# Attention in block turns: two tiles normalised by ScalarE, and the second pair's q and k loaded in four parts

## The chip, the cores and the metric

One core of one Trainium2 chip runs the whole program. The metric is the device time of one execution in microseconds. The kernel before took 1048.01 us in the median of three runs (1047.76 to 1048.04).

## The reference, cut to what matters

Attention with a position bias is followed by two mixture stages. The change lies in the attention alone.

```
scores = q @ k.T / sqrt(64)                       # 4 batches, 8 heads, 576 x 576
x      = log1p(|i-j|) / log1p(max(i,1))           # the bias stage:
bias   = relu(x * w1 + b1) @ w2                   # one 576 x 576 plane for each head
attn   = exp(scores + bias - max);  attn /= sum(attn)
out    = attn @ v                                 # then router, experts, gated FFN
```

## The kernel before, in words

**Bias stage** (`bias_stage`, up to about 65 us). Its 36 steps make 16 query rows each, for all 8 heads. In a step VectorE writes three hidden blocks (line 140) and ScalarE a fourth (line 234), TensorE multiplies them with w2 (line 267), ScalarE copies the product from PSUM into `b_res` (line 244), and SyncE (SP) stores these 288 KB to DRAM (line 151). `b_res` has four buffers: ScalarE's copy of step s waits until the store of step s-4 has landed (`s_st[u]`). On the same SP queue, `loads` issues other transfers at given steps, behind the store of the step: four tiny ones at steps 2, 4, 6 and 8; q and k of the second pair of heads, 576 KB each, both at step 22 (`load_qk(e, 1, 1)`); and two small ones at steps 28 and 30. At steps 10, 18, 26 and 34 SP loads a finished 576 KB tile of the bias back from DRAM (`load_bias`, line 331), after waiting for the stores that wrote it (line 155).

**Attention** (about 64 to 312 us). It runs over 16 pairs of heads. A pair has five slots: slots 0 to 3 hold 128 query rows of either head (h = 0, 1), slot 4 (`MIX`) the last 64 rows of both. For each unit TensorE makes the scores (line 437), VectorE adds the bias and takes the maximum (`add_bias`, line 597), ScalarE takes the exponential with its row sums (line 663), VectorE transposes it in blocks of 32 (`turn`, line 609). One slot later TensorE multiplies with v in four visits (`values`, line 552). ScalarE copies the finished output of a pair out of PSUM (`keep_out`, lines 671 and 677); TensorE turns it back into rows (`turn_back`, line 566), two pairs late, into the PSUM banks of the h = 1 scores; VectorE multiplies it by the reciprocals of the sums (`normal`, line 628), in two halves: tiles 0 and 1 (128x288), then tiles 2 to 4 (128x432). GpSimd adds up the router's part of that (line 508), SP stores the rest.

The order on each engine is written out by hand. In slot 3 of pair p VectorE does: `add_bias` of slot 4, both halves of `normal(p - 2)`, the turns of h = 0 and h = 1; in slot 4: `add_bias` of the next pair's slot 0 for h = 0 and h = 1, the turn of slot 4. TensorE does in slot 3: scores of slot 4, `turn_back(p - 2)`, the last visit of `values(p - 1)`; in slot 4: scores of the next pair's slot 0, h = 0 and h = 1. The scores of h = 1 wait for `s_x`, the semaphore that both halves of `normal` raise, because `turn_back` had used their banks. The pairs 2 to 13 run in a loop of six rounds with two pairs each, the others are written out; in the loop, waits for values that depend on the round need register instructions, and `sem.apart` puts an increment of a spare semaphore (line 87) between such waits.

Of the kernel before, what the change touches and what calls it, by code (L numbers as in the profile page):

```python
# [33 lines left out]
class Sems:  # L34
# [3 lines left out]
    LOOPS = """b_mm b_ev b_st0 b_st1 b_st2 b_st3 a_st00 a_st01 a_st10 a_st11 a_s a_b a_e a_t a_o a_oe a_bk a_r a_x a_pa  # L38
# [237 lines left out]
def front_stages(sem, arena, psum, qt, kt, vt, ww, wg, biasd, xd, ident, rt, small):  # L276
# [35 lines left out]
    s_s, s_b, s_e, s_t, s_o, s_oe, s_bk, s_r, s_x = (  # L312
        sem.loop("a_" + n) for n in ("s", "b", "e", "t", "o", "oe", "bk", "r", "x"))
# [40 lines left out]
    def split_k(e, it, u):  # L354

        pair = it * 2 + u
        e.wait_ge(s_k[u], sem.at(s_k[u], it * 16 + 16))
# [67 lines left out]
    def scores(e, p, u, uses, s, h):  # L425
# [4 lines left out]
        if s == 0 and h == 1 and from_pair(p, 3):  # L430
            e.wait_ge(s_x, sem.at(s_x, p * 2 - 4))
# [13 lines left out]
    def sync(e):  # L445

        def store_first(p, u):
            e.wait_ge(s_x, sem.at(s_x, p * 2 + 1))
# [5 lines left out]
        def store_second(p, u):  # L454
            e.wait_ge(s_x, sem.at(s_x, p * 2 + 2))
# [78 lines left out]
    def tensor(e):  # L534
# [54 lines left out]
    def vector(e):  # L589
# [11 lines left out]
        def turn(p, u, s):  # L601

            unit, n, w = p * TPP + 2 * s, p * SLOTS + s, (u + s) % 2
            if s == 0:
                e.wait_ge(s_o, sem.at(s_o, p - 1))
            for h in range(1 if s == MIX else 2):
                at = P if s == MIX else (P + Q) * h + Q * s
                e.wait_ge(s_e, sem.at(s_e, unit + h + 1))
                t = e.transpose(pt[:, u, :, at:at + Q], pr[:, w, S * h:S * h + S].rearrange("p (k q) -> p k q", q=Q))  # L609
            t.then_inc(s_t, 1)  # L610
# [7 lines left out]
        def normal(p, u, uses, half):  # L618

            n = 2 + half  # L620
            at = (slice(None), u, slice(2 * half, 2 * half + n), slice(None))
            if half == 0:
                e.wait_ge(s_r, sem.at(s_r, p * 2 + 2))
            st = (s_st0, s_st1)[half][u]
            e.wait_ge(s_bk, sem.at(s_bk, p * 2 + half + 1))
            e.wait_ge(st, sem.at(st, uses * (32, 64)[half]))
# [22 lines left out]
        for half in range(2):  # L649
            normal(NPAIR - 2, 0, NPAIR // 2 - 1, half)  # L650
        inverse(NPAIR - 1, 1)
        for half in range(2):
            normal(NPAIR - 1, 1, NPAIR // 2 - 1, half)

    def scalar(e):

        def exps(p, u, uses, s, h):
# [7 lines left out]
            mm.then_inc(s_e, 1)  # L665

# [1165 lines left out]
```

## Time and profile before

| | us |
|---|---|
| median of three runs | 1048.01 |
| the profiled execution | 1048.78 |
| its span, first to last instruction | 1046.9 |
| TensorE busy | 993.2 (95%) |
| VectorE busy | 791.9 (76%) |
| ScalarE busy | 410.0 (39%) |
| GpSimd busy | 203.8 (19%) |

Busy is the time in which an engine executes; the rest of the span it waits. The profiled execution is 0.77 us above the median of the runs, and its span 1.88 us shorter than its own time. Most of the time lies behind the attention, in stages that the change does not touch.

### The profile page before, as it was taken

What the parts mean: (1) busy time and instruction counts of PE and PEld (TensorE: products, weight loads), DVE (VectorE), ACT (ScalarE), POOL (GpSimd) and SP (SyncE); (2) the same over time, 40 slices, a digit from 0 to 9 for tenths busy, and PEclk for the clock granted to TensorE, in tenths of its full rate; (3) what the DMA queues carried; (4) which work ended last, traced back from release to release, by engine and by line L of the source; (5) the groups of instructions that cost most, each with busy time, mean ns of one, the idle gap of its engine ahead of it and who ended that gap; (6) DMA issues with size and microseconds to landing.
All of it is one profiled execution on the core that took longest, in us unless ns stands there. A gap on an engine that the chain in (4) does not pass through costs nothing.

```text
span 1046.9 us, 28553 instructions
## 1 busy us (share of the span) xinstructions
PE 993.2 (95%) x10409; PEld 901.3 (86%) x10410; DVE 791.9 (76%) x1268; ACT 410.0 (39%) x783; POOL 203.8 (19%) x195
## 2 busy tenths in 40 slices
PE   5868899999988999999999999999999999999997
PEld 2347788777877999999999999999999999999996
DVE  8978899999958457757474699787777767777675
ACT  6865555555534346444352352222111121211111
POOL 2035545655502212212120000000100100100101
PEclk9978999999999999999999999999999999999999
DMA  3874757758426816515122620020100100000000
GB/s 136 274 268 196 243 176 245 252 169 284 132 65 203 300 44 213 213 53 212 37 81 69 221 73 1 1 58 26 60 0 13 47 0 30 30 0 0 31 1 31
DMA packets 66797, 117.42 MB, mean 112 GB/s; under 512 B 27104, under 2 KB 38416, under 8 KB 64704
## 3 DMA queue, kind: packets, MB, share of 16 engines
q1 hardware_dynamic: 62720, 103.45, 29.3%
q0 software_dynamic: 4032, 13.37, 3.7%
q8 instruction: 28, 0.46, 0.2%
q14 instruction: 17, 0.14, 0.0%
HBM read 91.41 MB, written 25.40 MB: 112 GB/s over the span
## 4 chain that ended last, share of the span: by engine, by line
PE 68%; DVE 2%; issue 1%; POOL 1%; ACT 1%; DMA 0%; POOLq 0%; DVEq 0%
PE psum L1704 28%; PE psum L1712 14%; PE psum L1217 11%; PE psum L1226 11%; PE psum L1203 1%; PE psum L552 1%; PE psum L437 1%; DVE f_eg L1659 0%; PE psum L1265 0%; PE psum L566 0%; DMA e_xin<-x_tokens,e_col 0%; PE psum L847 0%; DVE r_inq L962 0%; POOL e_xin L1169 0%; POOL e_col L1165 0%
## 5 line engine op out<-in xcount | busy, mean ns | idle before, releaser
L1659 DVE RECIPROCAL f_eg<-f_eg 128x384 f32<-128x384 f32 x72 | 183.4, 2547 | 0.0
L1627 ACT ACTIVATE f_eg<-psum 128x384 f32<-128x384 f32 x72 | 35.5, 492 | 311.9 <-PE psum L1704 311.9
L663 ACT ACTIVATE a_pr<-a_sc,a_nmax 128x576 f32<-128x576 f32 x144 | 110.8, 770 | 96.3 <-DVE a_nmax L597 96.2
L1704 PE MATMUL psum<-f_x,f_ghi 128*128 (+1 forms) x576 | 147.6, 337 | 0.4 <-DVE f_x L1520 0.4
L1704 PE MATMUL psum<-f_x,f_vhi 128*128 (+1 forms) x576 | 146.1, 334 | 0.0
L597 DVE CUSTOM_DVE_ANT_0 a_sc<-psum,a_bias 128x576 f32<-128x576 f32 x144 | 104.3, 752 | 22.7 <-PE psum L437 20.2
L437 PE MATMUL psum<-a_khi,a_qs 128*128 128x288 f32 x320 | 101.1, 336 | 13.8 <-DVE a_nmax L597 13.8
L1704 PEld LDWEIGHTS psum<-f_x,f_ghi 128*128 128x128 f32 x576 | 105.8, 188 | 6.6 <-DVE f_x L1520 0.6
L1596 POOL DMA_INDIRECT out<-f_ob,f_cols x18 | 18.2, 1009 | 464.9 <-ACT f_ob L1613 316.9
L552 PE MATMUL psum<-a_pt,a_v 32*64 32x128 f32 (+1 forms) x4608 | 98.9, 294 | 8.3 <-issue 8.3
L1704 PEld LDWEIGHTS psum<-f_x,f_vhi 128*128 128x128 f32 x576 | 104.0, 188 | 0.0
L609 DVE STREAM_TRANSPOSE a_pt<-a_pr 128x576 f32<-128x576 f32 x144 | 103.9, 756 | 0.0
L1704 PE MATMUL psum<-f_x,f_glo 128*128 (+1 forms) x288 | 97.1, 337 | 0.0
L552 PEld LDWEIGHTS psum<-a_pt,a_v 32*64 32x64 f32 x4608 | 79.6, 131 | 20.1 <-issue 17.9
L1704 PE MATMUL psum<-f_x,f_vlo 128*128 (+1 forms) x288 | 96.2, 334 | 0.0
L1655 DVE TENSOR_SCALAR f_eg<-f_eg 128x384 f32<-128x384 f32 x72 | 26.5, 368 | 88.5 <-ACT f_eg L1627 88.5
L437 PEld LDWEIGHTS psum<-a_khi,a_qs 128*128 128x128 f32 x320 | 62.4, 195 | 34.6 <-DVE a_nmax L597 17.9
L437 PE MATMUL psum<-a_klo,a_qs 128*128 128x288 f32 x320 | 90.9, 304 | 0.0
L1226 PE MATMUL psum<-e_hhi,e_w2hi 128*128 128x288 f32 x288 | 87.4, 303 | 0.0
L1217 PE MATMUL psum<-e_xhi,e_w1hi 128*128 128x288 f32 x288 | 87.1, 303 | 0.0
L1712 PE MATMUL psum<-f_ohi,f_alo 128*128 128x512 f32 x216 | 85.4, 396 | 0.0
L1712 PE MATMUL psum<-f_olo,f_ahi 128*128 128x512 f32 x216 | 85.3, 395 | 0.0
(235 smaller groups left out, 2150.0 us busy)
## 6 DMA issues: line engine op xcount, KB each, us to landing
a_v<-v SPq DMA_DIRECT2D x16, 1152.0 KB, 5.6
e_raw<-ew SPq DMA_DIRECT2D x16, 1024.0 KB, 5.7
bias_ihj<-b_res SPq DMA_DIRECT2D x36, 288.0 KB, 2.6
a_qraw<-q SPq DMA_DIRECT2D x16, 576.0 KB, 4.4
a_kraw<-k SPq DMA_DIRECT2D x16, 576.0 KB, 5.4
a_bias<-bias_ihj SPq DMA_DIRECT2D x16, 576.0 KB, 6.5
xn_t<-e_yn SPq DMA_DIRECT2D x8, 576.0 KB, 3.1
x_tokens<-a_xp SPq DMA_DIRECT2D x64, 64.0 KB, 3.8
```

What stands on the lines that cost most here:

```text
L437: mm = e.matmul(s_ps[:, h, half, 0:HALF], qs[:, u, c:c + P], k[:, u, a * S + half * HALF:a * S + (half + 1) * HALF], start=(i == 0), stop= ...
L552: mm = e.matmul(o_ps[64 * h:64 * h + 64, g, to:to + n], vv[rows, u, k, 64 * h:64 * h + 64], pt[rows, u, k, first:first + n], start=(k == 0 ...
L597: e.tensor_tensor_reduce(sc[:, h, :].rearrange("p (a s) -> p a s", a=2), s_ps[:, h, :, 0:HALF], bias[:, 2 * s + h, :].rearrange("p (c s) - ...
L609: t = e.transpose(pt[:, u, :, at:at + Q], pr[:, w, S * h:S * h + S].rearrange("p (k q) -> p k q", q=Q))
L663: mm = e.activation(pr[:, w, S * h:S * h + S], sc[:, h, :], ACT.Exp, bias=nmax[:, h:h + 1], scale=-1.0, accum_out=sums[:, u, 2 * s + h:2 * ...
L1217: mm = e.matmul(bank[:, 0:BT], w[:, k, :], x[:, u, k, :], start=(k == 0 and n == 0), stop=(k == KD - 1 and n == 2))
L1226: mm = e.matmul(banks.y[:, k, 0:BT], w[:, k * P:(k + 1) * P], h[:, f % 3, :], start=(f == 0 and n == 0), stop=(f == KF - 1 and n == 2))
L1627: e.activation(self.eg[:, k % 2, :], self.g_ps[k % 2][:, 0:CHUNK], ACT.Exp, scale=-1.0).then_inc(self.s_e, 1)
L1655: e.tensor_scalar(x, x, 1.0, None, ALU.add).then_inc(self.s_c, 1)
L1659: e.reciprocal(x, x).then_inc(self.s_c, 1)
L1704: mm = e.matmul(acc[:, 0:CHUNK], a, b, start=(q == 0 and i == 0), stop=(q == KD - 1 and i == 2))
L1712: mm = e.matmul(self.o_ps[t], x, y, start=(f == 0 and i == 0), stop=(f == KFF - 1 and i == 2))
```

## The change

1. `normal` is split between two engines. ScalarE does tiles 0 and 1 as four copies with a scale, one for each tile and head (128x72 each), in slot 3 ahead of the exponential of slot 4. VectorE does tiles 2 to 4 as before, but between the turn of h = 0 and the turn of h = 1 of slot 3; `turn` takes the head as an argument for this. Both reciprocals of `inverse` are kept.
2. `s_x` becomes two semaphores, `s_xf` (ScalarE's part) and `s_xs` (VectorE's). Whoever waited for `s_x` now waits for one or for both: the scores of h = 1 of slot 0 on TensorE, with two more `sem.apart`; `turn_back`; the stores on SP; `add_logits` on GpSimd.
3. In the bias stage q and k of the second pair are loaded in four parts of 288 KB: the halves of k at steps 12 and 14, the halves of q at steps 16 and 20. The waits for them count 32 instead of 16 in the first round.

```diff
-        if step == 22:
-            load_qk(e, 1, 1)
+        if step in (12, 14, 16, 20):
+            i = (12, 14, 16, 20).index(step)
+            part = slice(S * (i % 2), S * (i % 2) + S)
+            if i < 2:
+                e.dma_start(kraw[:, 1, part], kt[1, :, part]).then_inc(s_k[1], 16)
+            else:
+                e.dma_start(qraw[:, 1, i % 2, :], qt[1, :, part]).then_inc(s_q[1], 16)
...
         if s == 0 and h == 1 and from_pair(p, 3):            # TensorE, scores
-            e.wait_ge(s_x, sem.at(s_x, p * 2 - 4))
+            e.wait_ge(s_xf, sem.at(s_xf, p - 2))
+            sem.apart(e, p)
+            e.wait_ge(s_xs, sem.at(s_xs, p - 2))
+            sem.apart(e, p)
...
                 if exists(np_) and ns != MIX:                # VectorE, pair
                     add_bias(np_, nu, nuses, ns, 1)
+                turn(p, u, s, 0)
                 if s == MIX - 1 and from_pair(p, 2):
-                    for half in range(2):
-                        normal(p - 2, u, uses - 1, half)
-                turn(p, u, s)
+                    normal(p - 2, u, uses - 1)
+                if s != MIX:
+                    turn(p, u, s, 1)
...
+        def normal(p, u, uses):                              # ScalarE
+
+            e.wait_ge(s_r, sem.at(s_r, p * 2 + 2))
+            e.wait_ge(s_bk, sem.at(s_bk, p * 2 + 1))
+            e.wait_ge(s_st0[u], sem.at(s_st0[u], uses * 32))
+            e.wait_ge(s_pa, sem.at(s_pa, p - 1))
+            for t in range(2):
+                for h in range(2):
+                    n = 2 * t + h
+                    x = e.activation(xp[:, u, t, h, :], back_ps[0][:, XW * n:XW * n + XW], ACT.Copy, scale=rinv[:, u, n:n + 1])
+            x.then_inc(s_xf, 1)
...
                 np_, nu, nuses, ns = next_of(p, u, uses, s)  # ScalarE, pair
+                if s == MIX - 1 and from_pair(p, 2):
+                    normal(p - 2, u, uses - 1)
                 if s == MIX and from_pair(p, 1):
                     keep_out(p - 1)
```

## Rows read from the trace of the kernel before

**Rows 1.** Page, parts 1 and 4: busy time, and the chain that ended last.

```profile
PE 993.2 (95%) x10409; PEld 901.3 (86%) x10410; DVE 791.9 (76%) x1268; ACT 410.0 (39%) x783; POOL 203.8 (19%) x195
...
PE 68%; DVE 2%; issue 1%; POOL 1%; ACT 1%; DMA 0%; POOLq 0%; DVEq 0%
```

**Rows 2.** Timeline of VectorE in two pairs: start us, us, instruction [idle before].

```profile
183.91 0.74 DVE L609 STREAM_TRANSPOSE a_pt<-a_pr 128x576 f32<-128x576 f32 x1
184.77 0.76 DVE L597 CUSTOM_DVE_ANT_0 a_sc<-psum,a_bias 128x576 f32<-128x576 f32 x1
...
196.25 0.76 DVE L597 CUSTOM_DVE_ANT_0 a_sc<-psum,a_bias 128x576 f32<-128x576 f32 x1 [0.63 <-PE psum L437]
...
197.92 1.43 DVE L609 STREAM_TRANSPOSE a_pt<-a_pr 128x576 f32<-128x576 f32 x2
199.37 0.76 DVE L597 CUSTOM_DVE_ANT_0 a_sc<-psum,a_bias 128x576 f32<-128x576 f32 x1
...
200.73 0.77 DVE L609 STREAM_TRANSPOSE a_pt<-a_pr 128x576 f32<-128x576 f32 x1
```

**Rows 3.** Timeline of TensorE in the same two pairs.

```profile
184.04 0.30 PE L437 MATMUL psum<-a_klo,a_qs 128*128 128x288 f32 x1
...
195.80 1.39 PE L566 MATMUL psum<-a_xw,a_ot 128*128 x10
...
198.63 0.30 PE L437 MATMUL psum<-a_klo,a_qs 128*128 128x288 f32 x1
...
199.16 0.29 PE L437 MATMUL psum<-a_klo,a_qs 128*128 128x288 f32 x1
...
201.89 0.40 PE L552 MATMUL psum<-a_pt,a_v 32*64 32x160 f32 x8 [0.23 <-issue]
```

**Rows 4.** Groups by line and shape, 110 to 300 us: busy, mean ns | idle.

```profile
L628 DVE TENSOR_TENSOR a_xp<-psum,a_rinv 128x432 f32<-128x432 f32 x13 | 7.8, 603 | 0.2
...
L677 ACT ACTIVATE a_ot<-psum 64x64 f32<-64x64 f32 x26 | 5.5, 212 | 0.2
```

**Rows 5.** Timeline of ScalarE in the second of the two pairs.

```profile
197.12 0.78 ACT L663 ACTIVATE a_pr<-a_sc,a_nmax 128x576 f32<-128x576 f32 x1 [1.79 <-DVE a_nmax L597]
...
198.39 0.60 ACT L671 ACTIVATE a_ot<-psum 128x512 f32<-128x512 f32 x1 [0.39 <-PE psum L552]
```

**Rows 6.** ScalarE in the bias stage: waits (total, times, longest), then its timeline.

```profile
ACT b_res L244 <- DMA bias_ihj<-b_res: 5.4, 3, 4.5
...
34.49 0.74 ACT L244 ACTIVATE b_res<-psum,b_invp 128x576 f32<-128x576 f32 x1 [0.53 <-DMA bias_ihj<-b_res]
...
55.12 0.74 ACT L244 ACTIVATE b_res<-psum,b_invp 128x576 f32<-128x576 f32 x1 [4.55 <-DMA bias_ihj<-b_res]
```

**Rows 7.** Line 151, stores issued 14 to 28, at 29.4, 46 to 50.5 us.

```profile
DMA to landing us min/median/max: 2.1/2.1/2.2
...
DMA to landing us min/median/max: 4.9/4.9/4.9
...
DMA to landing us min/median/max: 7.2/8.0/8.9
```

**Rows 8.** Windows: length, busy us of each engine, PEclk, DMA share, GB/s.

```profile
29.00:36.00 7.00, 6.45 (x92) 2.44 (x90) 7.00 (x18) 6.47 (x11) 0.00 (x0) 1.00 0.87 292
36.00:40.00 4.00, 3.67 (x56) 1.30 (x48) 4.00 (x11) 4.00 (x7) 0.00 (x0) 1.00 0.59 226
40.00:56.00 16.00, 10.94 (x152) 3.89 (x144) 15.77 (x37) 11.13 (x18) 0.00 (x0) 1.00 0.86 273
...
71.00:73.00 2.00, 1.39 (x7) 1.04 (x5) 2.00 (x5) 0.94 (x4) 0.62 (x4) 0.50 0.45 114
```

**Rows 9.** Timeline of VectorE in the bias stage.

```profile
12.76 43.01 DVE L140 TENSOR_SCALAR b_hid<-b_table,b_shift 128x576 f32<-128x576 f32 x100
59.21 1.38 DVE L140 TENSOR_SCALAR b_hid<-b_table,b_shift 128x576 f32 x3 [3.44 <-PE psum L267]
```

**Rows 10.** Timeline of VectorE at the end of the attention.

```profile
312.18 0.61 DVE L628 TENSOR_TENSOR a_xp<-psum,a_rinv 128x432 f32<-128x432 f32 x1 [0.22 <-PE psum L566]
```

More of the change, by code:

```diff
@@ L37 @@
     START = 128
-    LOOPS = """b_mm b_ev b_st0 b_st1 b_st2 b_st3 a_st00 a_st01 a_st10 a_st11 a_s a_b a_e a_t a_o a_oe a_bk a_r a_x a_pa
+    LOOPS = """b_mm b_ev b_st0 b_st1 b_st2 b_st3 a_st00 a_st01 a_st10 a_st11 a_s a_b a_e a_t a_o a_oe a_bk a_r a_xf a_xs a_pa
                e_xs e_xt e_xh e_xl e_h e_hh e_hl e_o e_sq e_yc e_pre e_ss e_rt e_inv e_ys e_st e_fold
@@ L311, in front_stages @@
     s_sp, s_kk, s_qh, s_ql, s_low = sem("a_sp"), sem("a_kk"), sem("a_qh"), sem("a_ql"), sem("a_low")
-    s_s, s_b, s_e, s_t, s_o, s_oe, s_bk, s_r, s_x = (
-        sem.loop("a_" + n) for n in ("s", "b", "e", "t", "o", "oe", "bk", "r", "x"))
+    s_s, s_b, s_e, s_t, s_o, s_oe, s_bk, s_r, s_xf, s_xs = (
+        sem.loop("a_" + n) for n in ("s", "b", "e", "t", "o", "oe", "bk", "r", "xf", "xs"))
     def load_qk(e, pair, u):
@@ L356, in split_k @@
         pair = it * 2 + u
-        e.wait_ge(s_k[u], sem.at(s_k[u], it * 16 + 16))
+        e.wait_ge(s_k[u], sem.at(s_k[u], it * 16 + 16 + 16 * u))
         sem.apart(e, it)
@@ L374, in split_q @@
         pair = it * 2 + u
-        e.wait_ge(s_q[u], sem.at(s_q[u], it * 16 + 16))
+        e.wait_ge(s_q[u], sem.at(s_q[u], it * 16 + 16 + 16 * u))
         sem.apart(e, it)
@@ L447, in store_first @@
         def store_first(p, u):
-            e.wait_ge(s_x, sem.at(s_x, p * 2 + 1))
+            e.wait_ge(s_xf, sem.at(s_xf, p + 1))
             sem.apart(e, p)
@@ L454, in store_second @@
         def store_second(p, u):
-            e.wait_ge(s_x, sem.at(s_x, p * 2 + 2))
+            e.wait_ge(s_xs, sem.at(s_xs, p + 1))
             sem.apart(e, p)
@@ L500, in add_logits @@
         def add_logits(p, u):
-            e.wait_ge(s_x, sem.at(s_x, p * 2 + 2))
+            e.wait_ge(s_xf, sem.at(s_xf, p + 1))
+            sem.apart(e, p)
+            e.wait_ge(s_xs, sem.at(s_xs, p + 1))
             sem.apart(e, p)
@@ L559, in turn_back @@
             e.wait_ge(s_oe, sem.at(s_oe, p + 1))
-            e.wait_ge(s_x, sem.at(s_x, p * 2))
+            e.wait_ge(s_xf, sem.at(s_xf, p))
+            e.wait_ge(s_xs, sem.at(s_xs, p))
             e.wait_ge(s_b, sem.at(s_b, min((p + 3) * TPP - 1, NPAIR * TPP) if isinstance(p, int) else (p + 3) * TPP - 1))
@@ L599, in add_bias, with turn @@
                                    -0.125, 3.0e38, ALU.add, ALU.min, nmax[:, h:h + 1]).then_inc(s_b, 1)
-        def turn(p, u, s):
+        def turn(p, u, s, h):
             unit, n, w = p * TPP + 2 * s, p * SLOTS + s, (u + s) % 2
-            if s == 0:
+            if s == 0 and h == 0:
                 e.wait_ge(s_o, sem.at(s_o, p - 1))
[L606 to L610, printed above, removed]
+            at = P if s == MIX else (P + Q) * h + Q * s
+            e.wait_ge(s_e, sem.at(s_e, unit + h + 1))
+            t = e.transpose(pt[:, u, :, at:at + Q], pr[:, w, S * h:S * h + S].rearrange("p (k q) -> p k q", q=Q))
+            if h or s == MIX:
+                t.then_inc(s_t, 1)
         def inverse(p, u):
@@ L616, in inverse @@
             e.reciprocal(rinv[:, u, TPP:TPP + 1], sums[:, u, TPP - 1:TPP]).then_inc(s_r, 1)
[L618 to L626, printed above, removed]
+        def normal(p, u, uses):
+            e.wait_ge(s_r, sem.at(s_r, p * 2 + 2))
+            e.wait_ge(s_bk, sem.at(s_bk, p * 2 + 2))
+            e.wait_ge(s_st1[u], sem.at(s_st1[u], uses * 64))
             e.wait_ge(s_pa, sem.at(s_pa, p - 1))
-            e.tensor_tensor(xp[at], back_ps[half][:, 0:2 * XW * n].rearrange("p (t h d) -> p t h d", t=n, h=2),
-                            rinv[:, u, 4 * half:4 * half + 2 * n].rearrange("p (t h) -> p t h", h=2)
-                            .unsqueeze(3).to_broadcast([P, n, 2, XW]), ALU.mult).then_inc(s_x, 1)
+            e.tensor_tensor(xp[:, u, 2:, :, :], back_ps[1][:, 0:6 * XW].rearrange("p (t h d) -> p t h d", t=3, h=2),
+                            rinv[:, u, 4:].rearrange("p (t h) -> p t h", h=2)
+                            .unsqueeze(3).to_broadcast([P, 3, 2, XW]), ALU.mult).then_inc(s_xs, 1)
         def pair(p, u, uses):
@@ L648, in vector @@
         each_pair(e, pair)
-        for half in range(2):
-            normal(NPAIR - 2, 0, NPAIR // 2 - 1, half)
+        normal(NPAIR - 2, 0, NPAIR // 2 - 1)
         inverse(NPAIR - 1, 1)
-        for half in range(2):
-            normal(NPAIR - 1, 1, NPAIR // 2 - 1, half)
+        normal(NPAIR - 1, 1, NPAIR // 2 - 1)
     def scalar(e):
@@ L665, in exps, with normal @@
             mm.then_inc(s_e, 1)
+        def normal(p, u, uses):
+            e.wait_ge(s_r, sem.at(s_r, p * 2 + 2))
+            e.wait_ge(s_bk, sem.at(s_bk, p * 2 + 1))
[6 more added lines that the diff above has]
+            x.then_inc(s_xf, 1)
         def keep_out(p):
@@ L692, in scalar @@
         each_pair(e, pair)
+        normal(NPAIR - 2, 0, NPAIR // 2 - 1)
         keep_out(NPAIR - 1)
+        normal(NPAIR - 1, 1, NPAIR // 2 - 1)
     def exp_table(e):
```

## The prediction, made before the changed kernel ran

> **What bounds the kernel now.** I read the page first. TensorE is busy 95% of the span and makes 68% of the chain that ended last; the other engines add a few per cent [rows 1]. So an edit pays only where TensorE itself waits, or where a stage is held up by something else. The change touches two places, and I read the timelines of both.
>
> *Attention, where pairs meet.* TensorE's last score matmul for h = 0 of the next pair's slot 0 starts at 198.63 and ends at 198.93 [rows 3]. VectorE's `add_bias` on it starts at 199.37 [rows 2], 0.44 us later. Which of the two held it, VectorE's turns or TensorE's scores? Here the turns end at 199.35, so VectorE looks busy to the end. The pair before answers it: its score matmul ends at 184.34 [rows 3] and `add_bias` starts at 184.77, 0.43 us later, although the turn had ended at 184.65 [rows 2]. The distance from TensorE is the same with and without a free VectorE. So `add_bias` is held by the scores, plus the register instructions behind its waits, and VectorE's turns end just inside that. From there the chain runs: two `add_bias`, the turn of slot 4 (200.73), the first `values` matmul at 201.89 [rows 2, 3], and then TensorE without a break to the same point of the next pair.
>
> *Bias stage.* ScalarE waits three times for a store of `b_res` to land, 5.4 us in all, 4.55 us of it at 55.12 [rows 6]. A quiet store lands 2.1 us after its issue; the one at 29.4, behind the tile load of step 10, took 4.9, the one behind q and k 8.9 [rows 7]. Landing time less stall is 4.4 us both times (4.9 - 0.5, 8.9 - 4.5). So a store may be 2.3 us late (4.4 - 2.1) at no cost, and all above it is a stall. What ScalarE loses here moves the start of the attention, for its exponentials wait behind the last `b_res`.
>
> **Part 1, `normal` on two engines.** On VectorE 14 pairs lose 0.45 us each between `add_bias` of slot 4 (196.25) and that of slot 0: normal now stands from 196.93 (196.25 and 0.68) to 197.92, afterwards it takes about 0.55 (the 128x432 form takes 0.60 [rows 4] and overlaps its follower). That is 14 x 0.45 = 6.3 us of busy time. But `add_bias` stays at 199.37, 0.44 behind TensorE, and TensorE in front of it (slot 4's scores, `turn_back` 195.80 to 197.19, `values`, scores) has no wait for VectorE in it. What is late next is what was late already. I take 0. The ends: 0, and 6.3 if the turns were the holder.
>
> On ScalarE four copies of 128x72 come ahead of slot 4's exponential. The nearest row is 0.21 us, for 64x64 out of PSUM [rows 4]; the far one is 0.60 for 128x512 [rows 5]. The first can start once the first four matmuls of `turn_back` are done, 195.80 + 4 x 0.12 + about 0.2 = 196.5, plus about 0.3 for its four waits: 196.8. With 0.21 each they end at 197.65, and the exponential starts there and not at 197.12, 0.5 late; it ends with its sums near 198.5. Queued behind it is `keep_out` (198.39), then 0.2 late; behind that the next pair's exponentials, which wait for `add_bias` of 199.37, so till 200.05, anyway. VectorE needs slot 4's exponential before `add_bias` at 199.37, whose waits must be over some 0.3 earlier, near 199.1: 0.6 to spare. Cost 0. It becomes a cost from 0.35 us a copy on; at 0.6 a copy it would be 1.0 us in each of 14 pairs, 14 us.
>
> TensorE's two more waits and increments stand between the scores of h = 0 and h = 1. VectorE's part of normal now runs after the turn of h = 0, about 197.6 to 198.2, before h = 1 needs the bank at 198.64. Should the queue cost 0.1 to 0.15, h = 1's scores end at 199.6 instead of 199.45 [rows 3]; their `add_bias` comes at 200.05. Cost 0, cover 0.3 us. The waits added to `turn_back` stand a microsecond ahead of it in the queue; those on SP and GpSimd belong to work that no one waits for inside a pair. At the end, VectorE's 128x432 half waited for the last `turn_back` matmul at 312.18 and not for the half before it [rows 10]. It does so still, and ScalarE does the other half beside it: 0.
>
> **Part 2, q and k in four parts.** A step of the stage takes 3 x 0.430 = 1.29 us (100 hidden blocks in 43.01 us [rows 9]). Prices in DMA time, mean over the 16 engines: from 36 to 40 us only three stores run, 0.59 x 4 / 3 = 0.78 us each, so a quiet step frees 0.5 us. From 29 to 36, 0.87 x 7 = 6.1, less five stores, leaves 2.2 for the 576 KB tile; from 40 to 56, 13.8 less nine stores leaves 6.8 for a tile, q and k, 2.3 each [rows 8]. The last engine sets the landing: the store behind the tile was 2.8 late with 0.5 freed, so a tile costs it 3.3; q and k together cost about 6.3.
>
> A part of 288 KB: by bytes half of 2.3 is 1.15, and half of the last engine's 3.2 is 1.6. The low end is the same 288 KB read in rows of the same length between 71 and 73 us with no stores beside it, 0.45 x 2 = 0.9 [rows 8]. The high end keeps the whole excess over moving the bytes: 3.2 - 1.5 + 0.75 = 2.45. I take 1.2, near the mean engine's price, since six reads in a row average the engines out.
>
> Now I walk the lateness of the stores, with 2.3 free, 0.5 freed each step: store 11 is 2.8 late (stall 0.5, as before). Each of the parts at 12, 14, 16 comes two steps after the last: 2.3 - 1.0 + 1.2 = 2.5, a stall of 0.2 each time. The tile at step 18 meets 1.8: 1.8 - 0.5 + 3.1 = 4.4, a stall of 2.1; the part at step 20 again 0.2. Sum 0.5 + 0.6 + 2.1 + 0.2 = 3.4, where it was 5.4; with the engines averaged over the tile too, 3.2. Gain 2.2 us. With 0.9 a part the stalls are about 2.3 (gain 3.1), with 1.6 about 4.9 (gain 0.5), with 2.45 about 8.3 (loss 2.9). Is VectorE then the bound? It stood idle 3.44 us for the stall before its last blocks [rows 9], so it can give back 3.4 and covers 2.2.
>
> The Trainium skill speaks against this edit: "DMA: Bandwidth & Descriptors", "Anatomy of one DMA", gives each DMA a fixed cost of about 2.0 us beside its bytes, and "Rules for kernel authors" there says to coalesce many small transfers into one large. By that, two more DMAs cost 4 us if it all fell on the engines, and the gain would be a loss of about 2. In the trace a quiet store needs 2.1 us to land but stores follow each other every 1.29 us at a share of 0.59 [rows 7, 8], so most of a fixed part overlaps; the range above does without the rule.
>
> **Sum.** 0 + (-2.2) = -2.2 us. The profiled execution's 1048.78 would become 1046.6; it stands 0.77 above the median, so against 1048.01 I expect 1045.8.
>
> **Rivals.**
> - *The stall stays* (22%). Each part pays the start of a read like a whole load (1.6 or more): stalls 4.9 to 6.3, time 1047.5 to 1048.9. For it: the excess of 0.8 to 1.7 us per load did not depend on what came before it. Against: the reads of 71 to 73 us had little of it.
> - *The stall goes* (12%). Spread out, the reads fall into the free 41% of 36 to 40 us; ScalarE could gain over 4, VectorE caps it near 3.9: 1044.1.
> - *VectorE held the pairs* (6%). Then 14 x 0.44 = 6.2 more: 1039.6. Against it is the pair at 184.77.
> - *ScalarE's copies are slow* (7%), the other side. Past 0.35 us a copy, the exponential of slot 4 comes after VectorE's wait for it. At 0.45 each, it is 0.4 x 14 = 5.6 us: 1051.4. For it: one copy per tile and head, each with its own fixed part; against: 0.21 for a like one.
>
> **How the numbers follow.** The forecast has 53%, with its own range 1044.8 to 1047.2. The predicted time is 1045.8. The range 1043.7 to 1048.8 takes in the first two rivals and most of the bounds of a part's price, and leaves out the last two. A change under 0.2% (2.1 us) can't be told from none here. My forecast stands at that edge: a little over half of its 53% lies beyond it, which with the stall gone and the VectorE rival makes faster 0.49; same is the rest of the forecast and most of the staying stall, 0.41; slower 0.10.
>
> **What would show it.** The waits of ScalarE on `bias_ihj<-b_res` total about 3.2 and not 5.4, none near 4.5, the longest at step 23; stores from step 12 on land in 4 to 6.5 us. VectorE waits 0.3 more for TensorE before `add_bias` of slot 0, the distance from the score matmul stays 0.43, and the time from one pair to the next stays. The copies take near 0.21 each. I am wrong if a pair gets shorter by 0.1 or longer, if the stall total is under 1.5 or over 4.5, or if the stages behind 312 us shift against each other.

## The result, and the profile after

The changed kernel took 1044.15 us (median of 6 runs, 1042.93 to 1044.45) beside 1047.88 for the kernel before (6 runs): ratio 0.9964, 95% interval 0.9951 to 0.9977. Forecast were 1045.8 us, ratio 0.9979, and a range of 1043.7 to 1048.8. The profiled execution took 1044.45 us with a span of 1042.6; that of before took 1048.78 with 1046.9.

The page: TensorE does the same work as in [rows 1]; VectorE has lost 7.3 us of busy time and ScalarE has gained 13.8.

```profile
PE 991.5 (95%) x10409; PEld 900.7 (86%) x10410; DVE 784.6 (75%) x1252; ACT 423.8 (41%) x847; POOL 206.2 (20%) x195
```

*Bias stage.* ScalarE's `b_res` rows with a wait, at steps 15, 23 and 31 (start us, us, instruction [idle before <- what ended it]). These answer to [rows 6]:

```profile
35.13 0.74 ACT L244 ACTIVATE b_res<-psum,b_invp 128x576 f32<-128x576 f32 x1 [0.46 <-DMA bias_ihj<-b_res]
...
47.03 0.74 ACT L244 ACTIVATE b_res<-psum,b_invp 128x576 f32<-128x576 f32 x1 [1.42 <-PE psum L267]
...
57.69 0.74 ACT L244 ACTIVATE b_res<-psum,b_invp 128x576 f32<-128x576 f32 x1 [0.19 <-PE psum L267]
```

The 4.55 us wait is gone, and together they are 2.1 us where three were 5.4. The second is put down to TensorE, but it is the store again: the one issued at 41.1, behind the tile of step 18, lands 5.8 us later, at 46.9, just ahead of the row. So is the third: the store of step 27, behind the tile of step 26, is issued at 53.0 and lands 4.5 us later. Issue to landing of the stores of line 151, issued 31 to 33.5 us, 33.5 to 39 us, and of that one:

```profile
DMA to landing us min/median/max: 4.2/4.3/4.4
...
DMA to landing us min/median/max: 2.8/3.6/3.8
...
DMA to landing us min/median/max: 5.8/5.8/5.8
```

The q and k reads now fill the room of [rows 8] (windows; the last two columns are DMA share and GB/s):

```profile
36.00:40.00 4.00, 3.64 (x56) 1.40 (x52) 4.00 (x10) 4.00 (x7) 0.00 (x0) 1.00 1.00 344
40.00:56.00 16.00, 13.17 (x188) 4.79 (x180) 16.00 (x39) 14.58 (x23) 0.00 (x0) 1.00 0.86 288
```

VectorE runs its hidden blocks without the 3.44 us of idle of [rows 9], and the attention's first `add_bias` follows at 61.26:

```profile
12.10 45.16 DVE L140 TENSOR_SCALAR b_hid<-b_table,b_shift 128x576 f32<-128x576 f32 x105
...
61.26 0.76 DVE L608 CUSTOM_DVE_ANT_0 a_sc<-psum,a_bias 128x576 f32<-128x576 f32 x1 [1.34 <-PE psum L445]
```

*Where pairs meet.* VectorE in the pair that answers to the second of [rows 2]:

```profile
192.68 0.76 DVE L608 CUSTOM_DVE_ANT_0 a_sc<-psum,a_bias 128x576 f32<-128x576 f32 x1 [0.62 <-PE psum L445]
...
194.06 0.57 DVE L635 TENSOR_TENSOR a_xp<-psum,a_rinv 128x432 f32<-128x432 f32 x1
194.55 0.76 DVE L619 STREAM_TRANSPOSE a_pt<-a_pr 128x576 f32<-128x576 f32 x1
195.81 0.76 DVE L608 CUSTOM_DVE_ANT_0 a_sc<-psum,a_bias 128x576 f32<-128x576 f32 x1 [0.50 <-PE psum L445]
```

Its turn ends at 195.31, and then it waits 0.50 us. From slot 4's `add_bias` to slot 0's it is 3.13 us; before it was 3.12 (199.37 - 196.25, [rows 2]). TensorE's last score matmul for h = 0 ends at 195.38, 0.43 ahead of `add_bias`, the distance of [rows 2, 3]:

```profile
195.08 0.30 PE L445 MATMUL psum<-a_klo,a_qs 128*128 128x288 f32 x1
```

ScalarE, against [rows 5]: four copies in 0.96 us, 0.21 apart (each lasts 0.32, overlapped), then the exponential.

```profile
193.07 0.96 ACT L682 ACTIVATE a_xp<-psum,a_rinv 128x72 f32<-128x72 f32 x4 [1.30 <-PE psum L577]
193.90 0.79 ACT L669 ACTIVATE a_pr<-a_sc,a_nmax 128x576 f32<-128x576 f32 x1
```

*Where the span's 4.3 us went.* Starts of a few instructions, us:

| landmark | before | after | difference |
| --- | --- | --- | --- |
| first `b_res` | 13.16 | 14.03 | +0.9 |
| first exponential of the attention | 65.66 | 63.03 | -2.6 |
| slot 4's `add_bias`, pair 3 | 121.87 | 119.36 | -2.5 |
| the same, pair 4 | 138.16 | 134.67 | -3.5 |
| the same, pair 14 | 282.75 | 278.92 | -3.8 |
| first `e_xin` (experts) | 334.95 | 331.38 | -3.6 |
| last `e_xin` | 573.30 | 568.99 | -4.3 |

2.6 us come in the bias stage, 1.0 between pairs 3 and 4, 0.35 in the ten pairs after that (0.3 are lost again on the way to the experts), 0.7 in the experts, where nothing was changed. What the last three are was the question for the experiments, beside the two parts of the change.

### The profile page after: what moved, and what is told of

Its sections match the earlier page's. It is cut to its first block, busy times and chain, and to the rows that moved or that the text cites. A ratio compares the mean times of both kernels' runs of the same rounds, so it can differ in the third digit from the quotient of the medians.

```text
span 1042.6 us, 28646 instructions
## 1 busy us (share of the span) xinstructions
PE 991.5 (95%) x10409; PEld 900.7 (86%) x10410; DVE 784.6 (75%) x1252; ACT 423.8 (41%) x847; POOL 206.2 (20%) x195
## 4 chain that ended last, share of the span: by engine, by line
PE 66%; DVE 2%; POOL 1%; issue 1%; DMA 0%; ACT 0%; POOLq 0%; DVEq 0%
PE psum L1726 28%; PE psum L1734 14%; PE psum L1239 11%; PE psum L1248 11%; PE psum L1225 1%; DVE f_eg L1681 0%; PE psum L1287 0%; DMA e_xin<-x_tokens,e_col 0%; DVE r_inq L984 0%; POOL e_xin L1191 0%; POOL e_col L1187 0%; PE psum L869 0%; PE psum L1231 0%; DVE f_alo L1669 0%; ACT f_ahi L1641 0%
## 5 line engine op out<-in xcount | busy, mean ns | idle before, releaser
L562 PE MATMUL psum<-a_pt,a_v 32*64 32x160 f32 (+1 forms) x4608 | 98.9, 297 | 8.2 <-issue 8.2
```

Of the source, the lines that this page charges most:

```text
L562: mm = e.matmul(o_ps[64 * h:64 * h + 64, g, to:to + n], vv[rows, u, k, 64 * h:64 * h + 64], pt[rows, u, k, first:first + n], start=(k == 0 ...
```

## The experiments

Each edit is against the kernel after, where nothing else is said. "Waits" are ScalarE's waits before `b_res` at steps 14 to 31, summed; "exp 0" is the start of the attention's first exponential, and "from 14" the us to it from the start of ScalarE's `b_res` of step 14. These come from one profile each, the ratio from the timed runs against the kernel before.

| kernel | waits | exp 0 | from 14 | median us | ratio (95%) |
| --- | --- | --- | --- | --- | --- |
| before, first and second profile | 5.4, 4.6 | 65.66, 66.00 | 33.2, 33.0 | 1047.0 to 1047.9 | 1 |
| after | 2.1 | 63.03 | 29.8 | 1044.15 | 0.9964 (0.9951 to 0.9977) |
| after, second time | 2.2 | 62.78 | 30.0 | 1045.71 | 0.9982 (0.9967 to 0.9997) |
| parts_only | 1.5 | 62.37 | 29.4 | 1043.69 | 0.9965 (0.9953 to 0.9977) |
| norm_only | 5.2 | 65.44 | 32.9 | 1048.98 | 1.0010 (0.9995 to 1.0026) |
| four_at_22 | 3.0 | 63.27 | 30.8 | 1047.26 | 0.9996 (0.9981 to 1.0011) |
| whole_12_16 | 2.9 | 63.30 | 30.8 | 1045.28 | 0.9976 (0.9962 to 0.9989) |
| spread_21_23 | 2.1 | 64.01 | 30.2 | 1045.31 | 0.9978 (0.9967 to 0.9990) |
| eight_pieces | 2.2 | 62.52 | 30.0 | 1045.09 | 0.9980 (0.9966 to 0.9994) |
| tile_in_halves | 0.25 | 61.42 | 28.6 | 1044.12 | 0.9977 (0.9962 to 0.9992) |
| after_dve_twice | 2.2 | 62.84 | 30.0 | 1044.83 | 0.9975 (0.9965 to 0.9986) |
| before_first_twice | 3.8 | 63.52 | 31.5 | 1048.48 | 1.0009 (0.9996 to 1.0022) |
| act_twelve | 2.1 | 61.68 | 29.8 | 1062.21 | 1.0134 (1.0116 to 1.0153) |

One and the same bias stage does not always give the same exp 0: it is 61.68 to 63.03 in the five profiles with the change's loads (after twice, parts_only, after_dve_twice, act_twelve) and 63.52 to 66.00 in the four with those of before. A part of that spread lies before step 14, where none of these kernels has yet waited for a store. From step 14 the five take 29.4 to 30.0 us and the four 31.5 to 33.2.

**Each part alone.** parts_only is the kernel before with the four loads and their waits (Part 2) alone; norm_only is the kernel after with

```
-        if step in (12, 14, 16, 20):
-            ...
+        if step == 22:
+            load_qk(e, 1, 1)
```

> The kernel before with only the second part of the change: q and k of the second pair in four parts at steps 12, 14, 16 and 20; VectorE still norms all five tiles. Theory (the bias stage gives the whole gain, the split of normal nothing inside a pair): ScalarE's DMA stalls in the bias stage near 1.9 us in place of 5.4, the attention's first exponential 2.6 us earlier than before, distance from pair to pair as before; time 2.5 to 3.5 us under before. Rival (the split of normal gives about 1 us of the gain through the pairs or the tail): only 1.5 to 2.5 us under before. Rival (the four parts alone do nothing, the gain is elsewhere): as before within 0.5 us.

> The kernel after with q and k whole at step 22 again: only the first part of the change. Theory: stalls in the bias stage 5.4 us as before, pair to pair as before, the one place that can move is the place near pair 4 where TensorE fetched code (1 us shorter after the change) and the expert stage (0.75 shorter); time as before to 1.5 us under it. Rival (VectorE's shorter work is worth 0.1 us or more in each of 14 pairs): 1.4 us or more under before, shown by a shorter distance from pair to pair. Rival (ScalarE's copies cost something in a pair that the bias stage's gain hid): slower than before by 0.5 us or more.

parts_only is as fast as the whole change. norm_only is not faster: its wait at step 27 is back, and its ratio puts it 1.0 us above before, with no change inside the interval. So its last rival, a cost of 0.5 us or more, has its number met but is not shown, and its pairs are not longer (below). The rows (ScalarE, parts_only first, then norm_only):

```profile
46.43 0.74 ACT L244 ACTIVATE b_res<-psum,b_invp 128x576 f32<-128x576 f32 x1 [1.34 <-DMA bias_ihj<-b_res]
```

```profile
54.92 0.74 ACT L244 ACTIVATE b_res<-psum,b_invp 128x576 f32<-128x576 f32 x1 [4.47 <-DMA bias_ihj<-b_res]
```

The split of `normal` gives nothing, and the bias stage all. The rival with 0.1 us a pair falls. Pairs 9 to 10 and 11 to 12 are 14.61 and 14.59 us long before and in parts_only 14.61 and 14.60, in after 14.45 both: there the split does give about 0.15. But in other profiles with the split the same two are 14.50 and 14.55 (norm_only), 14.46 and 14.54 (after, second time); it comes in some of the even pairs only and makes 0.35 us in ten pairs, too little for the timed runs to tell. The profiles settle it better once the places that differ from one execution to the next are taken out (last table of this section): norm_only then stands at 997.6 us beside 997.5 and 997.3 of before, and parts_only at 993.8 beside 994.0 of after both times.

**Splitting or spreading.** four_at_22 issues the four parts together; whole_12_16 spreads whole loads; eight_pieces halves each part; spread_21_23 moves two parts behind the tile.

```
four_at_22:    -        if step in (12, 14, 16, 20):      +        if step == 22:  (all four parts)
whole_12_16:   +        if step == 12: k of pair 1 whole  +        if step == 16: q of pair 1 whole
eight_pieces:  +        if step in (12, 13, 14, 15, 16, 17, 20, 21):  (S // 2 columns each)
spread_21_23:  +        if step in (12, 14, 21, 23):
```

> The kernel after, its four parts all issued at step 22, behind one another on SyncE's queue. It tells the splitting from the spreading. Theory (what counts is how much is read within a few steps; a DMA more costs little): the last store of the bias stage behind them lands as in before, 8 to 9 us after its issue, stall 4.5 to 5.0 us there, time 2.5 to 3.5 us over after. Rival (smaller DMAs share the engines better with the stores, so splitting alone removes the stall): stall under 2.5 us, time as after within 0.7 us. Rival (each DMA has a fixed price on the engines of about 1 us): stall 6 us or more, time over before.

> The kernel after with k whole (576 KB) at step 12 and q whole at step 16, no parts: spreading without splitting. The run with four parts at step 22 had stalls of about 3 us in its profile and a median time as before, so splitting alone gave little. Theory (bytes per step count, the number of DMAs hardly): stalls total 1.9 to 3.5 us, the largest 1.5 to 2 behind a whole load, first exponential 1 to 2.6 us before that of before, time 0 to 1.5 us over after. Rival (a whole load pays its start on the slowest engine, 3.2 us as in before, and the prediction's prices hold): lateness 4.5 at step 12 and 3.5 at 16, stalls 0.5 + 2.2 + 1.2 + 2.1 = 6.0 us, time as before or up to 1 us over it.

> The kernel after with its four parts at steps 12, 14, 21 and 23 in place of 12, 14, 16 and 20: a version that may beat both. In after, the one large stall (1.4 us) belongs to the store of step 19, 5.8 us from issue to landing, behind the tile load of step 18, with a part one step after it. Theory (a part next to the tile makes that stall): with the part at 16 and the one at 20 moved behind it, the store of step 19 lands in 4.9 to 5.4, stall 0.5 to 1.0 there, total 0.9 to 1.3, time 0.6 to 1.0 us under after. Rival (the parts at 21 and 23 hold the last stores, which gate the first exponential): stalls at steps 26 and 27, total 2 us or more, time as after or above. Rival (VectorE takes over as the bound of the stage): the stalls shrink but the first exponential stays within 0.3 us.

> The kernel after with each part halved again: eight of 144 KB at steps 12 to 17, 20 and 21, the same bytes over about the same steps with four DMAs more. Theory (the number of DMAs costs little beside the stores, the bytes per step count): stalls 1.5 to 2.5 us, time within 0.7 us of after. Rival (each DMA has a price of its own on the queue's engines; the prediction had 1.2 us for a part, of which its bytes are 0.75): four more at 0.45 are 1.8 us more lateness, stalls near 3.5, time 1.5 to 2 us over after. Rival (smaller pieces fit better between the stores): stalls under 1.2 us, time 0.5 us or more under after.

ScalarE's longest wait in each: four_at_22, whole_12_16 (two), spread_21_23, eight_pieces.

```profile
52.75 0.74 ACT L244 ACTIVATE b_res<-psum,b_invp 128x576 f32<-128x576 f32 x1 [2.71 <-DMA bias_ihj<-b_res]
```

```profile
38.93 0.74 ACT L244 ACTIVATE b_res<-psum,b_invp 128x576 f32<-128x576 f32 x1 [2.06 <-DMA bias_ihj<-b_res]
...
47.48 0.74 ACT L244 ACTIVATE b_res<-psum,b_invp 128x576 f32<-128x576 f32 x1 [0.67 <-DMA bias_ihj<-b_res]
```

```profile
58.32 0.74 ACT L244 ACTIVATE b_res<-psum,b_invp 128x576 f32<-128x576 f32 x1 [1.71 <-DMA bias_ihj<-b_res]
```

```profile
46.64 0.74 ACT L244 ACTIVATE b_res<-psum,b_invp 128x576 f32<-128x576 f32 x1 [1.96 <-DMA bias_ihj<-b_res]
```

Spreading whole loads takes the waits from about 5 to 2.9 us (1.9 to 3.5 expected); four parts at one step take them to 3.0, which my theory had not expected (it said 4.5 to 5.0 there). Both together give 2.1. So each half of the edit is worth some 2 us of wait in these single profiles (1 to 2.5, for before_first_twice, with the loads of before, had 3.8 us of waits) and the two overlap. The time of four_at_22 does not show its part, nor the 2.5 to 3.5 us over after that were expected: its runs spread from 1043.3 to 1050.0 us, and no gain and 2 us of gain are both inside the interval. Twice as many DMAs cost nothing (2.2 us of waits; 1045.09 us, beside 1045.71 for after timed with it). The Trainium skill, "DMA: Bandwidth & Descriptors", "Anatomy of one DMA", which describes DMAs issued from GpSimd (these are SP's), says of its fixed cost that completion latency makes most of it. By that most of it would not be time of the engines, and this run agrees: four more DMAs at 2 us each would have been 8 us, and the waits did not move. The rule to coalesce, which the prediction weighed, did not decide here.

spread_21_23 was meant to beat after and did not. The store of step 19 had little left to wait for (0.23 us), and the stall came back eight steps later, behind the next tile: the parts at 21 and 23 had used up the lateness that the tile of step 26 needs. With the same sum of waits as after, the first exponential comes 1.0 us later; 0.6 of that was there at step 14 already (33.80 and 33.22), so the edit's own part is 0.4.

**The tile in halves.** What is left in after is the wait behind the tile load of step 18.

```
+        if step == 20:
+            e.dma_start(bias[:, 3, :], biasd[P:2 * P, 1, :]).then_inc(s_bias[1], 16)
-        if step in (12, 14, 16, 20):
+        if step in (12, 14, 16, 22):
...
+        elif s == 1 and isinstance(hp, int) and hp == 0:
+            e.dma_start(bias[:, 2, :], biasd[P:2 * P, 0, :]).then_inc(s_bias[1], 16)
...                                                  # add_bias of slot 1 waits for 16 more
```

> The kernel after with the bias tile of step 18 in two halves, at steps 18 and 20, and the last part of q at step 22: a version that may beat both. The one stall of over a microsecond that is left in after belongs to the store of step 19 behind this tile. Theory (576 KB at once behind a store is what makes it late): that store lands in 4.4 to 5.0 us, stall 0 to 0.6 there, total 0.5 to 1.2, first exponential 0.8 to 1.4 us earlier than after, time as much lower. Rival (the store of step 19 is late by what came before it, not by the tile): stall 1.2 or more, time as after. Rival (VectorE or TensorE bounds the stage by now): the stall shrinks, the first exponential moves less than 0.4.

ScalarE's only wait left between steps 14 and 31, then the first exponential, and the landing of the five stores of steps 17 to 21, issued 37.7 to 42.9 us (in after their median is 5.2 and the longest 5.8):

```profile
55.42 0.74 ACT L244 ACTIVATE b_res<-psum,b_invp 128x576 f32<-128x576 f32 x1 [0.25 <-DMA bias_ihj<-b_res]
...
61.42 0.78 ACT L673 ACTIVATE a_pr<-a_sc,a_nmax 128x576 f32<-128x576 f32 x1 [0.55 <-DVE a_nmax L612]
```

```profile
DMA to landing us min/median/max: 3.3/3.8/3.9
```

The stall behind the tile of step 18 is gone and exp 0 comes at 61.42, 1.4 to 1.6 us before the two profiles of after. That alone would show little, for act_twelve, with the bias stage of after, has 61.68. But from step 14 it is 28.6 us beside 29.4 to 30.0 in the five profiles with the loads of after, 1.1 less than their mean: the theory is met. The waits are 1.8 us less, and not all of that arrives: the exponential now waits 0.55 us for VectorE, which the last rival had named. In time it is the fastest of the three kernels timed together (1044.12, beside 1045.71 for after), but the intervals overlap widely, so the stage's gain is seen, in one profile, and the kernel's is not. (Its span less the three hops of the last table is 991.9 us beside 994.0.)

**VectorE's room.** One more instruction like the changed one ahead of it, into a scratch tile: in after_dve_twice the 128x432 one, in before_first_twice the 128x288 one of the kernel before.

```
+            e.tensor_tensor(more[...], back_ps[...] ..., rinv[...] ..., ALU.mult)
             e.tensor_tensor(xp[...], back_ps[...] ..., rinv[...] ..., ALU.mult).then_inc(...)
```

> The kernel after; VectorE's normal of three tiles has one more instruction of the same size in front, into a scratch tile: about +0.55 us of VectorE work in each of 14 pairs between two add_bias. Theory (add_bias of slot 0 is held 0.43 to 0.44 us behind TensorE's score matmul, and the change gave VectorE some 0.45 us of room there): 0.0 to 0.1 us a pair, time within 1.5 us of after. Rival (VectorE's turns hold add_bias, so the room is not there): 0.5 us a pair, 7 us over after.

> The kernel before; VectorE's norm of the first two tiles has one more instruction of the same size in front, into a scratch tile: about +0.45 us in each of 14 pairs, at the place from which the change took it. Theory (before, the turns end just inside TensorE's gate, 0 to 0.15 us of room): 0.3 to 0.45 us a pair, 4 to 6 us over before, with add_bias of slot 0 now 0.75 to 0.9 us behind the score matmul. Rival (there was room of half a microsecond or more, VectorE was never near): within 1 us of before.

VectorE in pair 8 of after_dve_twice:

```profile
190.68 0.76 DVE L609 CUSTOM_DVE_ANT_0 a_sc<-psum,a_bias 128x576 f32<-128x576 f32 x1 [0.62 <-PE psum L446]
...
192.06 0.57 DVE L636 TENSOR_TENSOR a_more<-psum,a_rinv 128x432 f32<-128x432 f32 x1
192.55 0.59 DVE L639 TENSOR_TENSOR a_xp<-psum,a_rinv 128x432 f32<-128x432 f32 x1
193.07 0.76 DVE L620 STREAM_TRANSPOSE a_pt<-a_pr 128x576 f32<-128x576 f32 x1
193.80 0.76 DVE L609 CUSTOM_DVE_ANT_0 a_sc<-psum,a_bias 128x576 f32<-128x576 f32 x1
```

and of before_first_twice, with TensorE's last score matmul for h = 0 at the end:

```profile
194.35 0.76 DVE L598 CUSTOM_DVE_ANT_0 a_sc<-psum,a_bias 128x576 f32<-128x576 f32 x1 [0.62 <-PE psum L438]
...
195.03 0.45 DVE L630 TENSOR_TENSOR a_more<-psum,a_rinv 128x288 f32<-128x288 f32 x1
195.40 0.96 DVE L633 TENSOR_TENSOR a_xp<-psum,a_rinv 128x288 f32<-128x288 f32 x2
...
197.63 0.72 DVE L598 CUSTOM_DVE_ANT_0 a_sc<-psum,a_bias 128x576 f32<-128x576 f32 x1
```

```profile
196.74 0.30 PE L438 MATMUL psum<-a_klo,a_qs 128*128 128x288 f32 x1
```

In the first, slot 4 to slot 0 is 3.12 us, as without the added 0.5: it just filled the 0.50 us of idle, cost 0. In the second it is 3.28 and not 3.12: of 0.37 us added (195.40 - 195.03), 0.16 came through, so before the change VectorE had about 0.2 us of room, a little more than my theory here (0 to 0.15). `add_bias` stands 0.59 us behind the score matmul (197.63 - 197.04) and not 0.43; 0.75 to 0.9 had been expected. A pair got 0.13 us longer (mean of pairs 4 to 14: 14.59 us and 14.46), 1.9 us in 14 pairs; the ratio says +1.0 (-0.4 to +2.3), so the 4 to 6 us expected did not come. Together the two runs show that part 1 took 0.45 us of work out of a place in which VectorE was not the holder.

**ScalarE's room.** act_twelve:

```
+            for i in range(8):
+                e.activation(more[:, i, :], back_ps[0][:, XW * (i % 4):XW * (i % 4) + XW], ACT.Copy, scale=rinv[:, u, i % 4:i % 4 + 1])
             for t in range(2):
                 ...
```

> The kernel after; ScalarE makes eight more copies of 128x72 (into a scratch tile) ahead of its four, 12 in place of 4 in each of 14 pairs: +1.7 us of ScalarE at 0.21 us each. The prediction gave ScalarE 0.6 us of room ahead of slot 4's exponential (a cost from 0.35 us a copy on). Theory: 1.7 - 0.6 = 1.1 us a pair, 15 us over after. Rival (room of a microsecond, since the exponential of slot 4 is needed later than the prediction said): 0.5 to 0.7 us a pair, 7 to 10 us. Rival (no room was left by the change): 1.7 us a pair, 24 us.

ScalarE in pair 8, then VectorE and TensorE in the same pair, then two windows, each one pair long (us, busy of the engines, PEclk, DMA share, GB/s):

```profile
201.28 1.81 ACT L681 ACTIVATE a_more<-psum,a_rinv 128x72 f32<-128x72 f32 x8 [1.31 <-PE psum L578]
202.93 1.01 ACT L685 ACTIVATE a_xp<-psum,a_rinv 128x72 f32<-128x72 f32 x4
203.74 0.86 ACT L670 ACTIVATE a_pr<-a_sc,a_nmax 128x576 f32<-128x576 f32 x1
```

```profile
200.89 0.76 DVE L609 CUSTOM_DVE_ANT_0 a_sc<-psum,a_bias 128x576 f32<-128x576 f32 x1 [0.63 <-PE psum L446]
...
205.03 0.76 DVE L609 CUSTOM_DVE_ANT_0 a_sc<-psum,a_bias 128x576 f32<-128x576 f32 x1 [1.52 <-PE psum L446]
```

```profile
204.23 0.37 PE L446 MATMUL psum<-a_khi,a_qs 128*128 128x288 f32 x1 [0.66 <-ACT a_xp L685]
```

```profile
200.90:216.40 15.50, 13.76 (x340) 11.63 (x339) 13.21 (x30) 10.67 (x33) 7.91 (x5) 1.00 0.53 171
216.40:233.10 16.70, 15.26 (x340) 12.91 (x339) 13.26 (x30) 10.68 (x33) 7.90 (x5) 0.90 0.50 159
```

The exponential of slot 4 ends 3.71 us after slot 4's `add_bias` (204.60 - 200.89), in after 2.01 (194.69 - 192.68): 1.70 later. `add_bias` of slot 0 comes at 4.14 us and not at 3.13, so 1.01 later and again 0.43 behind what holds it, now the exponential. (Its row names TensorE, but the scores for h = 0 had ended at 203.57, 1.46 ahead; the exponential ended at 204.60.) Room in after: 1.70 - 1.01 = 0.69 us; the prediction had 0.6. The whole is 15.9 us a pair over pairs 4 to 14, 14.43 in after, so +1.5; in time it is 17.4 over after_dve_twice, whose time is that of after (1062.21 - 1044.83), more than the 15 expected. What I had not reckoned with is in the second window: TensorE's granted clock is 0.90 in the mean there, so part of the pair ran at the lower level (1.2 GHz), and 1.00 in the pair before, with the same instructions; the pair takes 1.2 us more (16.70 - 15.50). TensorE now waits for ScalarE's copies, 0.66 us in the row above, a wait that after does not have. It stands in both pairs (0.59 in the second), so why the clock fell in one of them and not in the other stays open.

**The rest of the difference.** Both kernels once more, unchanged.

> The kernel after, unchanged, a second profile and time beside the two below. So far the hops between landmarks of TensorE-bound pairs differed from profile to profile of kernels whose code is the same there: slot 4 of pair 1 to that of pair 2 took 16.0 or 17.5 us, pair 3 to 4 15.3 to 17.9. Theory (these are stalls of one execution, not of the change): the time is again 3 to 4 us under before, the bias stage's DMA stalls again 1.5 to 2.2, but the hops near pairs 1 to 4 differ from the first profile of after by 0.5 us or more somewhere. Rival (the shorter hop from pair 3 to pair 4 belongs to the change): it is 15.3 again here, and 16.3 in the unchanged kernel before.

> The kernel before, unchanged, a second profile. Theory: the stalls in the bias stage are 4 to 5.5 us again (5.4 in the first, 5.2 and 3.8 in two kernels with the same bias stage), the first exponential at 63.5 to 65.7, and the hops near pairs 1 to 4 differ from the first profile by 0.5 us or more somewhere. Rival: everything within 0.1 us of the first profile.

The hops between starts of slot 4's `add_bias`, from the first `e_xin` to the last, the span, and the span less the three hops 1 to 2, 3 to 4 and 14 to 15, us:

| profile | pair 1 to 2 | pair 3 to 4 | pair 4 to 5 | pair 14 to 15 | experts | span | less the three |
| --- | --- | --- | --- | --- | --- | --- | --- |
| before | 17.53 | 16.29 | 14.45 | 15.55 | 238.35 | 1046.9 | 997.5 |
| before, second | 17.29 | 15.39 | 14.47 | 15.55 | 237.99 | 1045.5 | 997.3 |
| parts_only | 16.04 | 15.63 | 14.46 | 15.84 | 238.30 | 1041.3 | 993.8 |
| norm_only | 17.58 | 17.85 | 14.45 | 17.19 | 238.82 | 1050.2 | 997.6 |
| after | 17.59 | 15.31 | 14.47 | 15.66 | 237.61 | 1042.6 | 994.0 |
| after, second | 17.58 | 15.30 | 14.47 | 17.78 | 238.15 | 1044.7 | 994.0 |
| tile_in_halves | 15.73 | 17.03 | 14.45 | 17.37 | 237.35 | 1042.0 | 991.9 |

The unchanged kernel before has the hop of 15.39 too, so the 1.0 us between pairs 3 and 4 was not the change's. The second timing of after is 1.9 us under before and not the 3 to 4 expected. The hop from pair 4 to 5 repeats to 0.02 us; those at three places move by 1.9 to 2.6 us between executions. The sum of the three goes with the span: after's second profile has 50.66 us there and the first 48.56, 2.1 more, and its span is 2.1 us longer; norm_only has 52.62 and before 49.37, 3.3 more, and its span is 3.3 us longer. Without them the profiles fall into groups, as the last column shows: 997.3 to 997.6 with the loads of before, 993.8 to 994.0 with the four parts, with and without the split of `normal`. (Of the others, after_dve_twice has 993.2, whole_12_16 993.8, eight_pieces 994.4, four_at_22 994.9, spread_21_23 996.4 and before_first_twice 996.7; a difference under 1 us means nothing here either.)

Two things make these hops long. One is a wait of TensorE that nothing in the profile releases. TensorE near pair 4, norm_only first, then after:

```profile
125.10 1.27 PE L557 MATMUL psum<-a_pt,a_v 32*64 32x128 f32 x24 [1.76 <-issue]
```

```profile
121.40 0.77 PE L562 MATMUL psum<-a_pt,a_v 32*64 32x128 f32 x24 [0.41 <-issue]
```

The two stand at the same operation; in tile_in_halves the wait is 2.13 us, in before 1.02. What the sequencer waits for there no run shows. In both traces above the queue that the profile calls q8 instruction moves 16 KB in the 2 us ahead of the wait (from 122 to 123 us and from 119 to 120), which fits a wait for code but does not prove it.

The other is TensorE's granted clock. The windows from one slot 4's `add_bias` to the next: pair 1 to 2 in after and in parts_only, pair 14 to 15 in after and in its second profile (the column before the last two is the clock):

```profile
87.31:104.91 17.60, 14.71 (x332) 12.51 (x333) 12.63 (x30) 8.30 (x21) 7.56 (x4) 0.90 0.37 137
```

```profile
86.15:102.19 16.04, 13.15 (x332) 11.08 (x333) 12.54 (x29) 8.19 (x21) 7.56 (x4) 1.00 0.39 150
```

```profile
278.92:294.58 15.66, 13.91 (x340) 11.72 (x339) 13.06 (x30) 9.14 (x25) 3.56 (x19) 1.00 0.33 97
```

```profile
278.44:296.23 17.79, 15.46 (x340) 13.08 (x339) 13.15 (x31) 9.15 (x25) 3.55 (x19) 0.90 0.30 86
```

A clock of 0.90 in the mean means that part of the hop ran at the lower level (1.2 GHz). The same pair takes 1.6 us more so in the first two windows, and 2.1 in the last two, 0.6 of which is a longer wait without a releaser (1.99 us for 1.42). In every profile of the table the hops of 17 us and more stand at 0.90 and those under 16.5 at 1.00; only the 17.03 of tile_in_halves stands at 1.00, with the wait of 2.13 us in it. In both windows of pair 1 to 2 TensorE has one long wait, of 2.07 and 2.08 us, so why the clock fell in one of them stays open. By this the long hops of norm_only (0.90 at all three places) and of after's second profile are chance and not the edit's.

The first `b_res`, at 14.0 in after both times, is at 13.2 in parts_only and 13.2 in eight_pieces and 14.0 in four_at_22, so that 0.9 us too belongs to an execution and not to an edit.

## Why the prediction was right, point by point

- *What bounds the kernel.* `add_bias` of slot 0 is held by TensorE's scores, 0.43 us behind: shown by after (distance unchanged, VectorE 0.50 idle) and by both doubled runs.
- *Part 1, 0 us.* Right: norm_only at 1.0010, parts_only as fast as after, and the same in the spans less the three hops. A few even pairs are about 0.1 shorter, which I had at 0; 0.35 us in all. The copies are 0.21 apart as taken, and the exponential has 0.69 us to spare (0.6 predicted). The idle before slot 0's `add_bias` became 0.50 us and not 0.3. The rival of VectorE holding the pairs is out; that of slow copies has the right mechanism, the price was not met.
- *Part 2, the walk of the lateness.* Its order was right: the largest wait at step 23, behind the tile of step 18, 1.4 us (1.9 the second time) for 2.1 predicted; step 15 at 0.46 for 0.5; a landing of 5.8 us with a wait of 1.4, so that 4.4 us is free as before. Mis-sized was the term of one part. At 1.2 us each of the four was to make the store behind it 0.7 us later than the one before it (1.2 less the 0.5 freed) and to add 0.2 us of wait; all four added 0. Behind the parts of steps 12 and 20 the landing goes from 4.2 to 4.4 us and from 5.2 to 5.4, which by the same reckoning is a part of 0.6 to 0.7 us; behind that of step 16 it goes from 2.8 to 3.8, a part of 1.5; the one of step 14 stands behind the wait of step 15 and can't be read so. (The landing of 5.4 cost no wait because the stall at step 23 had put off the copy that needed it.) The low bound of 0.9 was misread too: the reads of 71 to 73 us were two of 144 KB, and 0.23 MB of their 0.29 moved in that window. The excess over the bytes, which I gave to each read, does not come with each DMA: eight pieces cost no more than four. The walk had nothing at step 31, where the tile of step 26 made 0.19. Waits are 2.1 us against 3.2 to 3.4 predicted, and the stage gives 2.6 us and not 2.2 (first exponential, mean of five profiles with the four parts and of four without: 62.5 and 65.2; from step 14 it is 2.9).
- *The sum.* -2.2 forecast; the first timing says -3.7 (ratio 0.9964), the second -1.9 (0.9982). The stage's own 2.6 us lies between, and the spans less the three hops say -3.5. That the second timing's 1045.71 sits on the forecast 1045.8 is luck: the kernel before had 1047.0 in that timing, and the gain of the stage was forecast too small. The 1.0 us near pair 4, and the 0.7 in the experts, which I had named as a sign of being wrong, differ between executions of one kernel, and the first profile of after happened to have the short ones. So that sign told of the execution and not of the change.
- *The rival in which the stall goes* was near. VectorE's hidden blocks already end 3.3 us earlier in after (57.26 for 60.59), the idle time that was its cover, while exp 0 gained 2.6; tile_in_halves then removed the wait as well. Its attention starts at 61.42, 4.4 us before the mean of the two profiles of before and 3.7 before that of the four with its loads, beside the cap of 3.4 in one place of the prediction and 3.9 in another; and there the first exponential does wait for VectorE.

## What to carry to other kernels

When a stage waits on ring buffers that are stored while other data is read, follow the lateness: what a store may be late for nothing, what each step frees, and what each read adds; then move and split the reads until none passes the free amount. After one such read has been dealt with, look for the next largest before moving on, here the tile behind which the wait stood; a read moved behind another just moves the wait. Taking work from an engine is worth only its part of the holder's time, and a run that does that work twice tells in one look how much room there is.

## What the runs showed of the hardware that was not expected

- The number of DMAs for the same bytes did not matter between four and eight (waits 2.1 and 2.2 us), while 576 KB in one read, with parts of q before and behind it, made the store behind it land in 5.8 us (6.3 the second time; 4.7 in before, with no parts near it) and in two reads two steps apart in 3.9 at most, with the DMA share at 0.97 from 40 to 56 us, where after has 0.86 (windows of tile_in_halves):

```profile
36.00:40.00 4.00, 3.67 (x56) 1.30 (x48) 4.00 (x11) 4.00 (x7) 0.00 (x0) 1.00 0.98 339
40.00:56.00 16.00, 14.56 (x204) 5.29 (x200) 16.00 (x38) 15.75 (x25) 0.00 (x0) 1.00 0.97 333
```

- The granted clock of TensorE differs between executions of one kernel at the same place: pair 14 to 15 of after had 1.00 in one profile and 0.90 in the other, 15.66 and 17.79 us. In act_twelve it fell in one of two pairs with the same wait of about 0.6 us for ScalarE, 1.2 us more.
- Idle time that the trace calls issue differs between executions too (0.41 to 2.13 us at one matmul near pair 4). The hops at the three places differ by up to 2.6 us, and single times of one kernel by 3 to 8 us. A gain of 1 us in a stage can be seen in a profile but not in twelve runs of the whole, and in a profile only when it is counted from a point behind the places that vary.
